# Attention and a mixing layer in one kernel: the rounding copies of roped queries and keys run on VectorE in place of ScalarE

## The reference

```python
q_rot, k_rot = rotate(q), rotate(k)          # x1*cos - x2*sin, x1*sin + x2*cos
scores = (q_rot @ k_rot.T) / sqrt(64)
attn = exp(scores - rowmax) / (rowsum + 1e-9)
attn_out = attn @ v                          # then heads side by side: x is (4, 576, 512)
h = x.transpose(0, 2, 1) @ U @ V             # U (576, 32), V (32, 576)
u = x + h.transpose(0, 2, 1)
out = u + relu(u @ w_ch1) @ w_ch2            # (512, 2048), (2048, 512)
```

## Time and profile before

| | |
|---|---|
| median of 3 runs | 798.92 us (798.64 to 800.2) |
| profiled execution, its own time | 799.79 us |
| its span, first to last instruction | 797.7 us |
| PE busy | 725.8 us (91%) |
| DVE busy | 373.0 us (47%) |
| ACT busy | 373.4 us (47%) |
| POOL busy | 260.1 us (33%) |

### The profile page before, as it was taken

One profiled execution on the slowest core, in us unless ns is written; L12 is line 12 of the kernel. 1 busy time (PEld: TensorE's weight loads), 2 busy tenths in 40 slices (PEclk: granted clock), 3 DMA queues, 4 the chain that ended last, 5 costly groups with the idle time before them and its releaser, 6 DMA issues.

```text
span 797.7 us, 11651 instructions
## 1 busy us (share of the span) xinstructions
PE 725.8 (91%) x4336; PEld 655.4 (82%) x4336; DVE 373.0 (47%) x619; ACT 373.4 (47%) x807; POOL 260.1 (33%) x182
## 2 busy tenths in 40 slices
PE   0799998989898989987499999999999999999998
PEld 0689887778787878775499999999999999999997
DVE  2689897788778897786411121121212112122112
ACT  1689998789878989774433211111210111111100
POOL 6667758556866658300455200000000000000000
PEclk9999999999999999999799999999999999999999
DMA  7856665577457753523763030011003003001001
GB/s 239 237 147 188 174 189 139 152 225 197 127 164 227 205 164 90 130 70 119 219 243 128 1 119 1 0 61 59 1 1 118 1 1 119 0 1 40 1 1 39
DMA packets 45942, 86.47 MB, mean 108 GB/s; under 512 B 7552, under 2 KB 20032, under 8 KB 43840
## 3 DMA queue, kind: packets, MB, share of 16 engines
q1 hardware_dynamic: 45456, 84.50, 35.9%
q10 hardware_dynamic: 432, 1.25, 0.4%
HBM read 43.25 MB, written 14.16 MB: 72 GB/s over the span
## 4 chain that ended last, share of the span: by engine, by line
PE 50%; DVE 1%; ACT 0%; issue 0%; DVEq 0%
PE ps L842 25%; PE ps L855 25%; DVE utl L802 1%; DVE res L809 0%; ACT wh L777 0%; DVE wl L813 0%; DVEq L808 0%
## 5 line engine op out<-in xcount | busy, mean ns | idle before, releaser
L819 DVE SCALAR_TENSOR_TENSOR htl<-ps,hth 128x384 fp32r<-128x384 f32 x96 | 53.5, 558 | 325.8 <-ACT hth L794 325.8
L794 ACT ACTIVATE hth<-ps 128x384 fp32r<-128x384 f32 x96 | 47.2, 492 | 328.1 <-PE ps L842 328.1
L496 DVE TENSOR_REDUCE negmax<-ps 128x1 f32<-128x576 f32 (+1 forms) x160 | 120.2, 751 | 55.1 <-PE ps L602 53.7
L602 PE MATMUL ps<-stack 128*128 128x288 f32 (+1 forms) x640 | 125.3, 319 | 22.3 <-DMA stack<-raw 22.3
L842 PE MATMUL ps<-uth,wh 128*128 128x384 f32 x384 | 130.1, 339 | 10.1 <-DVE utl L802 10.1
L412 ACT ACTIVATE prob<-ps,negmax 128x576 f32<-128x576 f32 (+1 forms) x160 | 118.4, 740 | 41.8 <-DVE negmax L496 40.9
L842 PE MATMUL ps<-uth,wl 128*128 128x384 f32 x384 | 130.0, 338 | 0.0
L842 PE MATMUL ps<-utl,wh 128*128 128x384 f32 x384 | 129.5, 337 | 0.0
L502 DVE TENSOR_TENSOR ptl<-ps,pth 128x512 fp32r<-128x512 f32 (+1 forms) x192 | 121.4, 646 | 3.6 <-ACT pth L421 1.9
L855 PE MATMUL ps<-wl,hth 128*128 128x512 f32 x288 | 114.0, 396 | 0.0
L620 PE MATMUL ps<-ident,prob 128*128 128x128 f32 (+1 forms) x672 | 97.7, 270 | 17.7 <-ACT prob L412 16.1
(11 more groups left out here) (65 smaller groups left out, 860.4 us busy)
## 6 DMA issues: line engine op xcount, KB each, us to landing
stack<-raw SPq DMA_DIRECT2D x192, 144.0 KB, 2.6
raw<-in_qk SPq DMA_DIRECT2D x16, 1152.0 KB, 5.5
tables<-in_w SPq DMA_DIRECT2D x11, 512.0 KB, 4.5
raw<-scratch_ut SPq DMA_DIRECT2D x6, 768.0 KB, 6.7
res<-scratch_u SPq DMA_DIRECT2D x18, 256.0 KB, 3.5
out<-res SPq DMA_DIRECT2D x18, 256.0 KB, 2.1
vraw<-in_v SPq DMA_DIRECT2D x16, 256.0 KB, 5.3
scratch_u<-xn SPq DMA_DIRECT2D x16, 256.0 KB, 3.2
```

The lines of the kernel that those rows point to most:

```text
L496: nc.vector.tensor_reduce(negmax[0:w, n % NT:n % NT + 1], scores_of(n, w), AX.XY, ALU.max, negate=True).then_inc(maxed, 1)
L602: mm = nc.tensor.matmul(ps[0:w, at_:at_ + CH], stack[:, r % 2, i, 0, P * t:P * t + w], stack[:, r % 2, i, part, CH * c:CH * c + CH], start ...
L794: nc.scalar.activation(hth[:, i % 2], up_bank(i), ACT.Relu).then_inc(relu_hi, 1)
L819: nc.vector.scalar_tensor_tensor(htl[:, i % 2], up_bank(i), 0.0, hth[:, i % 2], ALU.max, ALU.subtract).then_inc(relu_lo, 1)
```

## The change

The 30 copies that the slot loop makes (for pairs 1 to 15, queries and keys) leave ACT's loop and stand in DVE's. In ACT they were after `round_p` of the slots s = 1 and s = 3; in DVE they are at the end of the same slots, after `split_p` and the mixing work and so in front of the next slot's `row_max`. They wait for the same semaphore (`roped`) and raise the same one (`qk_hi`). The two copies of pair 0, ahead of the loop, stay on ACT.

```diff
@@ scalar
-                if r + 1 < NPAIRS:
-                    if s == SPLIT_Q:
-                        split_qk(r + 1, 0)
-                    if s == SPLIT_K:
-                        split_qk(r + 1, 1)
-                    if s == SPLIT_V:
-                        split_v(r + 1)
+                if r + 1 < NPAIRS and s == SPLIT_V:
+                    split_v(r + 1)
@@ vector
+            def split_qk(r, which):
+                dve.wait_ge(roped[which], r + 1)
+                nc.vector.tensor_copy(raw[:, r % 2, 1, which].bitcast(F32R),
+                                      raw[:, r % 2, 0, which]).then_inc(qk_hi[which], 1)
+
             for n in range(SLOTS):
+                r, s = divmod(n, 2 * NT)
...
                 for item in mixes_of(n - 1):
                     mix(*item)
+                if r + 1 < NPAIRS:
+                    if s == SPLIT_Q:
+                        split_qk(r + 1, 0)
+                    if s == SPLIT_K:
+                        split_qk(r + 1, 1)
```

## The result

The changed kernel takes 811.68 us (median of 4 runs, 810.15 to 814.23) against 799.56 for the kernel before in the same session (4 runs, 798.64 to 800.86): a ratio of 1.0154, with a 95% interval of 1.0123 to 1.0184. It is 12.1 us slower. The forecast was 811 us.

A forecast was written before the change was run, and what follows sets the result against it. In the attention half, DVE's maximum, which each exponential waits for, was taken to be on the path. Delays of 13.2 us less 1.4 of ACT's relief gave about +12 over a median of 798.92, so 811 us (range 802 to 818).

The forecast's parts named there:

- Short and held: DVE's copy takes 0.42 us, but only after waiting for GpSimd's running instruction; the forecast's own case, 811 us, chance 0.50.
- Pairs 2 to 4: Query copy held by GpSimd's key rope; tile 4's exponential 1.2 us late in each pair, 3.6 us in all.
- Pairs 5, 9, 13: DVE waits for roped queries in ACT's place, then is held; 2.4 us a pair, 7.2 us in all.
- Pairs 6, 10, 14: Query copy hidden while DVE waits 3.01 us for scores, key copy costs 0.4 each; 1.2 us in all.
- Pairs 1, 8, 12: Query copy covered by DVE's hole of 0.72 us, key copy costs 0.4 each; 1.2 us in all.
- Pairs 7, 11: Query copy before a maximum waiting 0.52 us for scores, key copy delaying an exponential TensorE does not need yet; nothing.
- ACT's relief: ACT without its copies gives back 0.24 us a pair in pairs 1, 6, 8, 10, 12, 14; 1.4 us.
- Free and long: Rival: the DVE copy takes 0.66 us and GpSimd doesn't matter; 8.6 us more, 807.5 us; chance 0.20.
- Held and long: Rival: the DVE copy takes 0.61 us after each wait for GpSimd; about 18 us more, 817 us; chance 0.09.
- free and short: Rival: the DVE copy is short and not held by GpSimd; some 3.5 us more, 802.5 us; chance 0.05.
- Relief: Rival: ACT paces the attention half, so removing its copies brings back 4.7 us, 794 us; chance 0.11.
- Hidden: Rival: DVE's holes of 0.72 and 0.3 us take up both copies; 799 us; chance 0.05.

The follow-up runs named there:

- one-column form: The changed kernel with each DVE copy written as a maximum over a dimension of one element; 808.81 us against 798.57 for the kernel before, ratio 1.0127.
- 2 columns: The changed kernel with its own DVE copy over only the first 2 of 576 columns; 807.85 us against 799.53 for the kernel before, ratio 1.0096.
- keys alone: The changed kernel with only the fifteen key copies on DVE, query copies staying on ACT; 806.35 us, ratio 1.0094 to the kernel before.
- queries alone: The changed kernel with only the fifteen query copies on DVE, key copies staying on ACT; 810.59 us against 798.57 for the kernel before, ratio 1.0143.
- ropes-first kernel: The changed kernel with GpSimd's natural mixing subtractions three slots later, so ropes come first; 796.59 us against 800.41 for the kernel before, ratio 0.9968.
- ropes-first runs: GpSimd's natural mixing subtractions three slots later in the kernel before (788.95 us), the changed kernel (796.59) and the changed kernel with one-column copies (797.57).

## Why the prediction was right, step by step

- **What bounds the kernel.** Right. The maximum is what the exponential waits for, and ACT's copies lay beside it. ACT's waits for the maximum rose from 40.9 to 78.7 us. Totals of waits, the kernel before and the changed one:

```profile
ACT prob L412 <- DVE negmax L496: 40.9, 57, 7.6
```

```profile
ACT prob L412 <- DVE negmax L491: 78.7, 81, 7.6
```

- **Short and held.** Right, and shown: 451 ns for an instruction over 576 columns, a stretch to 1.33 to 1.38 us in pairs 2 to 4, gone with a one-column form and still there with 2 columns. It had been reasoned from four rows of the start, none of them a copy. One sign of it failed: the median over 1 us that the group was to show if held. It is 0.451, since 17 of the 30 copies, twelve of the fifteen key copies among them, meet no GpSimd instruction, and the maximum of 1.68 shows the hold. The Trainium skill's rule ("SBUF — State Buffer", Who interferes with whom), that such a copy and GpSimd exclude each other, agrees with these runs; its formula of 0.36 us ("VectorE: DVE Perf Modes", the TRN2 errata) is short of the 0.45 measured, and that page's fixed term of about 150 cycles, measured there on a bf16 copy of 2048 elements, gives an estimate of 0.46 for this one.
- **Pairs 2 to 4**: 3.6 forecast, 3.3 measured. Tile 2's exponential was forecast 1.35 us late; it came at 105.92 in place of 102.55, and 2.2 us of that were there when the pair began, so 1.15.
- **Pairs 5, 9, 13**: 7.2 forecast, 6.6 measured, 2.5, 2.6 and 1.6. By their first heads they are alike, 2.14, 1.95 and 2.16, against 2.4 forecast. The rest is the clock, which the prediction did not have: pair 13 gives 0.6 back in its second head, as it also does in the runs with keys alone, one column and two columns, because the fall in the kernel before cost it 0.7 there.
- **Pairs 6, 10, 14**: 1.2 forecast, 0.5 measured; the query copy lasts 1.67 us there and costs nothing. **Pairs 1, 8, 12**: 1.2 forecast, 0.9 measured.
- **Pairs 7, 11**: nothing forecast, 0.75 measured. This cover was misjudged. The run with queries alone loses nothing in these pairs and that with keys alone 0.74, so the key copy is the cause. It delays the DVE subtraction behind it, which frees the bank that TensorE needs for its next mixing transposes, which have no such wait in the kernel before. TensorE in the changed kernel:

```profile
179.85 0.66 PE L663 MATMUL ps<-ident,xn 128*128 128x128 f32 x4 [0.31 <-DVE ptl L497]
```

- **ACT's relief**: 1.4 us taken off, 0.24 in each of six pairs. Measured in the plain pairs: 0.1 us in all three pairs together. The control, the five slots without copies, was 0.24 us shorter for another reason, which stayed open. What relief there is lies in pairs 5, 9 and 13, where the forecast had none. Two errors of about 1 us, this and the sum of the parts at 13.2 in place of 12.1 (11.7, and 0.38 in pair 1), cancelled. The mechanism was right; that the forecast came within 1 us of the time is luck in part, the more so as the falls of the clock could have moved either kernel by as much.
- **The rivals.** "Free and long" would have given the same time: its own kernel took 808.8 us. The time could not tell it from the forecast, only the durations could. "Held and long" and "free and short" fell with the durations. "Relief" fell with the run in which ACT's copies shrink to two columns: 2.4 us at most. "Hidden" fell in the pairs with keys alone.

## What to carry to other kernels

Before an instruction goes to a less busy engine, look at what it stands in front of there: 20.5 us of copying left an engine that was 96% busy and took 1.4 to 2.4 us from the path at most, and came to stand before the one instruction that every tile waits for. A copy on DVE that stays within SBUF was short here (0.45 us), but it queued behind GpSimd as if it were one of GpSimd's instructions (up to 1.68 us); next to a busy GpSimd a longer form that is not held can cost the same. And a wait that all engines feel is best followed to its start: here it was one subtraction in GpSimd's order, worth nearly as much as the whole change cost. Where such a wait leaves TensorE idle, look at its granted clock in the stretch behind it before a difference is explained by the order.

## What the runs showed of the hardware that was not expected

The hold does not depend on width. The query copies of pairs 2 to 4 lasted 1.04 to 1.08 us with 2 columns and 1.33 to 1.38 with 576, and both groups differ by the same 0.3 us where nothing holds them (0.16 and 0.45). And taking turns, as the earlier trace rows and pair 5 show it, is not the rule: in the ropes-first kernel the copy was passed over by two GpSimd instructions that followed one another without a wait, 3.48 to 3.51 us in each of three pairs, though in pair 5 of the changed kernel it got in between L336 and L338. What decides this was not found out.

TensorE's granted clock fell after some of its idle times and not after others of the same length. In the kernel before it stood idle for 2.43 us in pair 5 and the clock stayed up; after 2.42 and 2.43 us in pairs 9 and 13 it fell. In the changed kernel it fell in all three after 4.17 to 4.19 us, but in the one-column kernel it stayed up in pair 13 after 3.28. In the loop order with the ropes first there is no such idle time, and no fall in these pairs in any of the three kernels. It is the same between 35 and 50 us: the kernel before and the one-column kernel both have TensorE idle up to 40.4 and 40.3 us, for 2.06 and 2.18 us, and only the first has the fall (the columns as in the earlier trace rows):

```profile
35.00:50.00 15.00, 12.58 (x84) 11.50 (x83) 12.62 (x21) 11.66 (x27) 10.44 (x8) 0.89 0.68 193
```

```profile
35.00:50.00 15.00, 12.16 (x90) 10.76 (x90) 13.93 (x24) 12.23 (x28) 11.64 (x8) 1.00 0.62 181
```

A mean of 0.89 means 1.2 GHz for part of the stretch. The exponential at 53.48 us came 1.0 to 1.9 us earlier in the runs without it. That is why the sums of the table start behind it. The falls also carry much of the scatter of one kernel's time: of the 23 executions of the kernel before that were measured beside the ropes-first runs, the three with a mean clock of 0.989 took 798.2 to 799.2 us, the twelve with 0.985 took 800.0 to 801.5. What decides whether the clock falls was not found out.
